# Two-part kernel on one core: weight blocks of the lead made in odd steps of four pairs and two at its end, row scales ahead of the norm's sum

## The reference

```
scores = q @ k.T / sqrt(64), causal          # 4 x 8 heads, 576 rows, 64 columns
local  = softmax(scores) @ v
phi    = elu(q) + 1                          # max(x,0) + min(exp(x),1)
mem    = (phi @ M_prev) / (phi @ z_prev + 1e-6)
attn   = g * mem + (1 - g) * local           # g = sigmoid(beta), one per head
x = attn as 2304 x 512
x = (sigmoid(x @ w_gate) * (x @ w_val)) @ w_out          # 512 -> 1536 -> 512
h = x @ w_in                                             # 512 -> 2048
out = (h * clip(h + 3, 0, 6) / 6) @ w_out2               # 2048 -> 512
```

## Time and profile before

| | |
|---|---|
| median of 3 runs | 1062.78 us |
| the profiled execution's own time | 1062.8 us |
| its span | 1061.0 us |
| PE, DVE, ACT, POOL busy over the span | 98%, 67%, 62%, 51% |
| granted TensorE clock | 1.0 throughout |
| lead, from the first matmul to the first product with `WG` | 8.41 to 91.59 us |

### The profile page before, as it was taken

One profiled execution on the slowest core, in us unless ns is written; L12 is line 12 of the kernel. 1 busy time (PEld: TensorE's weight loads), 2 busy tenths in 40 slices (PEclk: granted clock), 3 DMA queues, 4 the chain that ended last, 5 costly groups with the idle time before them and its releaser, 6 DMA issues.

```text
span 1061.0 us, 20622 instructions
## 1 busy us (share of the span) xinstructions
PE 1039.8 (98%) x6676; PEld 977.1 (92%) x6676; DVE 712.3 (67%) x1542; ACT 658.9 (62%) x1478; POOL 538.7 (51%) x584
## 2 busy tenths in 40 slices
PE   5999999999999999999999999999999999999998
PEld 4768999999999999999999999988989888988897
DVE  6986877877877877877745444765676655665553
ACT  5998777778777778877754433465556334543333
POOL 5997667568667668667536654168870101000000
PEclk9999999999999999999999999999999999999999
DMA  8553443443543442543223345344555444454411
GB/s 194 139 140 74 115 115 91 120 115 79 131 119 88 118 119 75 133 121 77 81 61 110 91 145 147 136 158 160 169 188 179 121 110 120 119 178 119 120 50 60
DMA packets 126350, 126.92 MB, mean 120 GB/s; under 512 B 12080, under 2 KB 92464, under 8 KB 126000
## 3 DMA queue, kind: packets, MB, share of 16 engines
q1 hardware_dynamic: 125968, 122.07, 41.6%
q10 hardware_dynamic: 288, 3.67, 0.9%
HBM read 106.30 MB, written 19.40 MB: 118 GB/s over the span
## 4 chain that ended last, share of the span: by engine, by line
PE 91%; ACT 3%; DVE 2%; issue 2%; POOL 1%; DMA 0%; SPq 0%; DVEq 0%; POOLq 0%; ACTq 0%
PE ps L834 87%; PE ps L878 4%; PE ps L891 1%; POOL prob L710 1%; ACT WG L1223 0%; DMA qk_st<-qk_t 0%; ACT h_gate L1386 0%; DVE Cb L1836 0%; DVE prob L1632 0%; ACT pt_hi L1195 0%; ACT L1240 0%; ACT L1386 0%; DVE h_val L1789 0%; ACT prob L1240 0%; DVE pt_lo L1572 0%
## 5 line engine op out<-in xcount | busy, mean ns | idle before, releaser
L834 PE MATMUL ps<-x_hi,WG 128*128 128x288 f32 x1536 | 322.0, 296 | 0.3 <-issue 0.2
L834 PEld LDWEIGHTS ps<-x_hi,WG 128*128 128x128 f32 x1536 | 250.6, 188 | 1.9 <-issue 1.3
L834 PE MATMUL ps<-x_lo,WG 128*128 128x288 f32 x768 | 226.2, 294 | 0.0
L834 PE MATMUL ps<-XC,WC 128*128 128x384 f32 x1008 | 202.3, 336 | 0.4 <-DVE Cb L1836 0.3
L834 PEld LDWEIGHTS ps<-XC,WC 128*128 128x128 f32 x1008 | 180.3, 188 | 15.6 <-issue 1.2
L673 POOL TENSOR_TENSOR WG<-stage,WG 128x512 fp32r<-128x512 f32 x96 | 124.7, 1318 | 92.7 <-ACT WG L1223 92.7
L834 PE MATMUL ps<-wo,G_hi 128*128 128x512 f32 x540 | 168.0, 392 | 0.0
L834 PE MATMUL ps<-h_hi,WO 128*128 128x288 f32 x768 | 164.8, 298 | 0.3 <-DVE Y L1809 0.2
L834 PEld LDWEIGHTS ps<-x_lo,WG 128*128 128x128 f32 x768 | 144.3, 188 | 0.5
L1836 DVE TENSOR_TENSOR Cb<-ps,Cb 128x384 f32<-128x384 f32 x168 | 89.0, 554 | 80.4 <-PE ps L834 79.0
L834 PEld LDWEIGHTS ps<-h_hi,WO 128*128 128x128 f32 x768 | 126.3, 188 | 1.5 <-DVE Y L1809 1.0
(11 more groups left out here) (143 smaller groups left out, 2053.2 us busy)
## 6 DMA issues: line engine op xcount, KB each, us to landing
WC<-w_in_parts SPq DMA_DIRECT2D x112, 256.0 KB, 2.7
stage<-w_out SPq DMA_DIRECT2D x64, 256.0 KB, 2.9
qk_st<-qk_t SPq DMA_DIRECT2D x54, 288.0 KB, 4.4
stage<-w_gate SPq DMA_DIRECT2D x48, 256.0 KB, 3.5
stage<-w_val SPq DMA_DIRECT2D x48, 256.0 KB, 2.9
w_in_parts<-WC SPq DMA_DIRECT2D x42, 256.0 KB, 2.0
qn_st<-q_n SPq DMA_DIRECT2D x16, 256.0 KB, 3.4
w_in_parts<-WC ACTq DMA_DIRECT2D x2, 1792.0 KB, 7.2
```

The costliest lines, as they stand in the source:

```text
L834: return pe.matmul(o, l, r, start=start, stop=stop, skip_group_check=True)
```

## The change

Four edits, in all five engines' lists but PE's, whose order stays as it was.

1. `first_block` gives block n in the step `(n, 1)` of pairs 0 to 3, and none in the steps `p = 0`. Blocks 4 and 5 come in pair 4: ScalarE rounds block 4 first thing in `(4, 0)` and block 5 in `(4, 1)` after the third exponential; GpSimd makes both rests at the end of `(4, 1)`.
2. The loads of blocks 3 to 6 are started in the steps `(1, 0)`, `(2, 0)`, `(3, 0)`, `(4, 0)`. Those of blocks 7 and 8 move from `(3, 1)` and `(4, 0)` into the first step after the lead, behind that step's loads of v, q and k.
3. On VectorE the row scales of the head of `(n, 0)` stand ahead of `phi_norms`, for pairs 1 to 4.
4. `phi_gates` moves from `(n, 1)`, where it stood behind the mask of the second tile, into `(n, 0)`, ahead of it.

```diff
         def first_block(n, p):
-            k = 2 * n + p - 2
-            return k if 0 <= k < GV else None
+            k, even = divmod(2 * n + p - 1, 2)
+            return k if not even and 0 <= k < FIRST else None
...
                 if r is not None:
+                    for k in (GV + 1, GV + 2) if isinstance(r, int) and r + p == 0 else ():
+                        stage_block(r, q, k)
                     for x, (ahead, k) in enumerate([x for slot in CUT[p] for x in slot]):
...
                 if n == FIRST and p == 1:
                     cut_v(n, 0)
+                    for k in (GV - 2, GV - 1):
+                        low_w(0, k)
...
                 if p == 0:
-                    block()
+                    if n == FIRST:
+                        high_w(0, GV - 2)
                     cut_q(n, 1)
...
                     second_tail(n, p)
-                    block()
+                    if old:
+                        block()
                     exp_tile(n, p, 1)
                     cut_q(n + 1, 0)
+                    if not old:
+                        block()
...
                     exp_tile(n, p, 2)
+                    high_w(0, GV - 1)
                     move_hi(n, p, "phi", 0, None)
...
-                    phi_norms(n)
                     if n >= 1:
                         row_scales(n, 1)
+                    phi_norms(n)
                     phi_inverses(n)
+                    if n >= 1:
+                        phi_gates(n)
                 elif n < FIRST:
                     if n >= 1:
                         mask_tile(n, p, 1)
-                    phi_gates(n)
                     if n == 0:
+                        phi_gates(n)
                         row_scales(n, p)
...
                     mask_tile(n, p, 1)
-                    phi_gates(n)
                     phi_scaled(n)
```

## The result

| | before | changed |
|---|---|---|
| median | 1062.51 us (1062.13 to 1062.98, 4 runs) | 1068.49 us (1066.74 to 1069.02, 4 runs) |
| ratio | | 1.0051, 95% interval 1.0038 to 1.0063 |
| profiled execution, span | 1062.8, 1061.0 | 1066.74, 1064.9 |

The change makes the kernel slower by 0.5%, 6 us by the medians and 4 by the profiled executions. The sign was forecast; the time lies outside the range (1060.7 to 1067.4).

What follows compares the result with a forecast made beforehand. The prediction took a ring of waits to pace the lead and PE to bound the kernel from 91.59 us on. Lead -1.3 plus PE's standstill +3.8 gave +2.5 us: span 1063.5, time 1065.3, range 1060.7 to 1067.4.

Steps and rivals of the forecast that it cites:

- The sign: Whole kernel: slower than before; chance 0.48 of slower by over 0.2%, 0.12 of faster, 0.40 within 0.2%.
- The sum: Whole kernel: -1.3 us for the lead plus 3.8 us for PE's standstill gives +2.5 us, time 1065.3.
- the stall: First step after the lead: PE stands 3.8 us because ACT waits for late loads of blocks 7 and 8; bounds 2.7, 4.7.
- The lead's gain: Stretch up to the first product with WG: 1.3 us sooner through edits 1, 3 and 4; bounds 0.3 and 4.1.
- PE is the bound behind G0: From the first product with WG, 91.59 us: PE busy 28.20 of 28.26 us, so gains or losses ahead reach the end.
- Pair 1 gives nothing: Lead, pair 1: its 1.1 us gain is spent on POOL's new block in (0, 1) and on PE, which sets that pair.
- the second and third turn: Lead, pairs 2 to 3 and 3 to 4: 0.8 and 0.6 us gained, 1.4 together.
- the slack of 0.95: After the lead, ACT may be late by 0.95 us at no cost: 0.75 slack plus a 0.2 wait that vanishes.
- Edit 4, forecast at nothing: Lead, VectorE: puts 0.4 us ahead of one mask and takes it away behind; the mask after next stays where it was.
- The third rival: Lead: POOL's scaled rows hold three VectorE instructions per pair; lead 0 to +0.5, standstill 3.8, time 1066.6 to 1067.1; chance 0.13.
- The rule that I had counted against edits 3 and 4: Lead: VectorE and GpSimd share a port pair as exclusive lock; the second comer is held for the other's whole instruction.
- this ring: Lead: waits among POOL, DVE, ACT and PE set the pace; no engine alone full, POOL busy 15.66 of 16.79 us.

Runs made afterwards that it cites:

- the loads-first kernel: Changed kernel with the loads of blocks 7 and 8 issued ahead of that step's v, q and k loads: 1060.45 us, ratio 0.9979; once more 1060.60 us.
- the late loads alone: Kernel before, with only the loads of blocks 7 and 8 moved behind the q and k load after the lead: 1070.42 us, ratio 1.0071.
- the repeat: The changed kernel run again, nothing altered, for a second profile: 1066.91 us, ratio 1.0043 to the kernel before.
- with PE kept busy: Changed kernel with 40 unused matmuls on PE in its wait after the lead: 1066.86 us, ratio 1.0034 to the kernel before.
- the slow orders: The loads-first kernel with phi_gates back behind the mask (1065.60 us), or with phi's scaling also ahead of the mask (1065.63 us).
- loads between: Changed kernel with the loads of blocks 7 and 8 between the v load and the q and k load: 1065.54 us, ratio 1.0025.

## Why the prediction was wrong

Two steps failed. The sum takes the standstill of PE for its whole cost, so the granted clock that follows it stands at nothing, without a reason; in V0 alone it measured 1.4 to 1.6 us in three profiles and 2.5 in a fourth. And the stall, 3.8 by the sum with 4.7 as its upper bound, measured 5.3. The lead's gain was sized too small the other way, which hid part of both.

Right: PE is the bound behind G0, and what is lost ahead of V0 stays lost. The lead's gain is smaller than what the loads of edit 2 cost, and their mechanism is the one predicted, from SyncE's issue over ACT's wait to G4's copy. Shown by the loads-first kernel, which removes wait, standstill and half clock together, and by the late loads alone, which bring all three back. Three sizes were off in the profiled execution: the lead by -1.2, the stall by +1.5 and the clock by +1.5 (which the sum did not have), and 1065.3 with these is 1067.1 for an execution of 1066.74 (0.2 of the rest is what PE had lost before on the way to V0). Without the third the time would lie within the range. That the repeat's median does so with all three is the luck of errors of opposite sign.

**The lead, -1.3 forecast.** The step that failed here is "Pair 1 gives nothing". Rows 0.86 after `q_exp` (0.90), POOL's wait of 0.7 after k_lo (0.73) and 9.0 from `q_exp` to `pt_lo` and G0 (G0 starts 9.8 after the last `q_exp` ends; before 9.6) came as said, and the second and third turn gained 0.8 and 0.8 where I had 0.8 and 0.6. But the turn from pair 1 to 2 gained 1.4. In the repeat of the changed kernel the five `q_exp` start at 13.80, 30.36, 46.23, 62.23 and 78.24; before at 13.70, 29.56, 46.86, 63.64, 80.42. Ahead of pair 1 it is 0.8 behind, about the 0.7 counted for POOL's new block, and then the turn is 15.87 instead of 17.30: PE does not hold that pair at its old length. The gain at G0 is 2.0 in this execution (89.58), and 2.5 in the profiled one of the result. All six other profiles whose PEclk is 0.50 from about 16 to 22 us are like the latter: their first scaled rows start at 18.3 to 18.6 us, where the rest have 18.9 to 19.0. By the rows it is not the half clock that gains this, since the passes of both kinds are at half pace from 16 to 22 us, but the passes at full pace from about 12 us up to it: VectorE's mask and `znorm_e` come sooner, and `znorm_e` takes 0.17 instead of the 1.16 of the repeat. This was read and not tried. The old lead varies as well: in the kernel with only the late loads, whose lead has the old order, `q_exp` of pair 1 is at 30.21 and G0 at 92.13, against 29.56 and 91.59. Against that profile the repeat is only 0.15 behind ahead of pair 1. The changed lead has G0 at 89.58 and, with PE kept busy, at 89.83 where the fast passes are missing, so without them the gain is 1.8 to 2.5 us.

**The stall, +3.8 forecast.** PE stood 5.3. Counted from G0's old start the two loads went out at 102.63 instead of 102.3 (100.11 + 2.52): 0.3. The second landed about 5.0 after its own issue instead of 4.2 (ACT done at 106.26 + 2.52 = 108.78, against my 107.65): 0.8. And the slack of 0.95 was 0.65: 0.3. 3.8 + 0.3 + 0.8 + 0.3 is 5.3 with the hundredths, the arithmetic of the earlier trace rows with three terms a little short. Both bounds of the stall (2.7 and 4.7) lie below it, and not because of the landing: 5.0 is within the 5.1 that I took for the longest. The bounds gave the issue and the slack no range, and these two are the 0.6 that is missing. An estimate by the fit of the Trainium skill ("DMA: Bandwidth & Descriptors", section "Anatomy of one DMA"), which it gives for loads issued by GpSimd, is 2.6 us for such a load; the 4.8 and 5.0 measured here behind v, q and k are far from it.

**The term that was missing.** The sum had no clock in it. A standstill of PE of 3.8 to 5.3 us was followed in all four profiles that have one by a granted clock of 0.50, for 3 or 6 us, at a price of 1.4 to 2.5 us. The profile of before shows no fall (from 20 to 92 us PE's longest idle piece is 1.64 us; the one of 2.46 ahead of 19.51 lies where the passes are at half pace anyway), but a sum that lets PE idle for several microseconds has to carry it in its range. The median of 1068.49 lies another 1.75 above the profiled 1066.74: the three other runs have a mean clock of 0.997, which fits the long half clock (+1.0, 5.65 against 4.66 for V0) without the fast passes near the start (+0.5). That is worked out from the means alone, and 0.25 of it is left over.

**Edit 4, forecast at nothing,** was judged wrongly. Taken away it costs 5.2 us with edit 3 in place and 0.8 without. The third rival (POOL's rows hold VectorE's norm work and each turn loses) describes what happens then, and edit 4 is what keeps it away. The rule that I had counted against edits 3 and 4, in the Trainium skill ("SBUF — State Buffer", section "Who interferes with whom"), agrees with `rsum_e` held for 1.05 to 1.33 us. But with the gates back it is `zscale` and phi's scaling that take 0.64 and 1.82 instead of 0.26 and 1.04, so read with that lock the rows speak for edit 4: what counts is which of POOL's instructions VectorE meets.

Left open: why the kernel with PE kept busy lost a microsecond to others far behind V0; why one standstill is followed by a short, a long or no half clock; whether the holds on VectorE in the slow orders are all of their turns of 17.2 and 17.3 us, which was read from the rows and not tried apart from the order; and why some executions have PE's passes at full pace from 12 to 16 us.

## What to carry to other kernels

When a change moves a load, find the first engine that will wait for it and count from issue to landing with what is queued ahead of it, and give every term of that count a range, the issue and the slack too and not the landing alone; then put the load ahead of the queue rather than behind it, which here turned +0.4% into -0.2%. If the sum lets PE stand for several microseconds, add the half clock that follows, 1.4 to 2.5 us here, as a range. Two profiles of one kernel differ by half a microsecond in the lead alone, so a gain of that size needs more than one. In this ring, where three engines are each 90% busy, the edits were not worth their own sum: test such edits together and apart, since the two on VectorE gave -2.0 us together, and -0.8 and +3.1 apart.

## What was not expected of the hardware

- The length of the half clock after nearly the same standstill (5.3 and 5.1 us): 3.2 us (changed kernel), about 6 (late loads only), and by the means of the runs sometimes none (loads between, 3.8 us of standstill, 1063.6 us).
- After the shorter standstill of 3.81 us the clock fell only after PE had run over 1 us at 1.00 again.
- 40 idle products in the standstill kept the clock at 1.00 in all five runs.
- A `tensor_tensor` of 128x640 on VectorE took 1.04 us when it started beside the last of POOL's four short rows and 1.82 us when it started behind it.
- PE's passes at half pace up to some 22 us in the profile of before, in stretches whose granted clock is given as 1.00.
